# A loop with an empty first pass around the experts' stage of a fused attention, experts and gated-product kernel

## The reference

```python
def attention(q, k, v, f_logit):            # (4, 8, 768, 48)
    f = 1 / (1 + exp(-f_logit))
    for t in range(768):
        state = f[t] * state + outer(k[t], v[t])
        y[t] = q[t] @ state

def experts(x, expert_emb, tau, w1, w2):    # 3072 tokens of 384, 8 experts, width 1024
    logits = unit(x) @ unit(expert_emb).T / tau
    e = argmax(logits, axis=1)
    return softmax(logits)[e] * (relu(x @ w1[e]) @ w2[e])    # per token, one expert

def gated_product(x, w_a, w_b, w_out):      # width 1536
    return ((x @ w_a) * (x @ w_b)) @ w_out
```

## Time and profile before

| | |
|---|---|
| median of 3 runs | 830.19 us (829.87 to 831.49) |
| profiled execution | 830.27 us |
| its span, first to last instruction | 829.0 us |
| TensorE busy | 810.1 us, 98% |
| VectorE, ScalarE, GpSimd busy | 364.4, 321.6, 141.1 us |
| mean granted TensorE clock | 0.995 |

### The profile page before, as it was taken

The page is one execution under the profiler, slowest core; times in us unless marked ns, Lnnn a source line. Parts: engine busy times, 40 slices in busy tenths (PEclk is TensorE's granted clock), DMA queues, the critical chain, the costliest instruction groups (busy, mean ns, idle before and its releaser), DMA issues.

```text
span 829.0 us, 14425 instructions
## 1 busy us (share of the span) xinstructions
PE 810.1 (98%) x5400; PEld 736.9 (89%) x5401; DVE 364.4 (44%) x597; ACT 321.6 (39%) x608; POOL 141.1 (17%) x206
## 2 busy tenths in 40 slices
PE   5999998989999999999999999999999999999998
PEld 4999987989999999998888888888888888888887
DVE  6788877836453645356532322232232223222221
ACT  5677775435453545355421321231222212212211
POOL 4544440423232322100000100010010001001001
PEclk9999999999999999999999999999999999999999
DMA  9777752556552554320000100010010001000001
GB/s 211 194 207 193 201 176 88 110 192 212 206 174 92 207 199 155 125 77 1 0 1 1 39 1 0 1 39 1 0 39 1 1 1 38 1 1 10 28 1 39
DMA packets 32572, 67.57 MB, mean 82 GB/s; under 512 B 12145, under 2 KB 21390, under 8 KB 31374
## 3 DMA queue, kind: packets, MB, share of 16 engines
q1 hardware_dynamic: 28174, 55.93, 22.0%
q0 software_dynamic: 4352, 11.04, 4.3%
HBM read 57.48 MB, written 9.48 MB: 81 GB/s over the span
## 4 chain that ended last, share of the span: by engine, by line
PE 97%; DVE 1%; issue 1%; DMA 0%; ACT 0%; POOL 0%; DVEq 0%
PE low_banks L1024 18%; PE scores L1024 18%; PE sums L1031 9%; PE high_banks L1031 9%; PE sums L978 8%; PE low_banks L967 6%; PE scores L967 6%; PE high_banks L978 4%; PE scores L812 3%; PE sums L828 3%; PE high_banks L801 2%; PE sums L819 2%; PE low_banks L787 2%; PE low_banks L795 1%; PE high_banks L839 1%; PE sums L901 1%
## 5 line engine op out<-in xcount | busy, mean ns | idle before, releaser
L568 POOL DMA_INDIRECT out<-out_sb,placed x24 | 23.3, 970 | 469.3 <-ACT out_sb L758 463.4
L1024 PE MATMUL low_banks<-x_hi,wab_lo 128*128 128x512 f32 x216 | 84.7, 392 | 0.0
L1024 PE MATMUL scores<-x_hi,wab_lo 128*128 128x512 f32 x216 | 84.7, 392 | 0.0
L1024 PE MATMUL low_banks<-yT_lo,wab_hi 128*128 128x512 f32 x216 | 84.6, 392 | 0.0
L1024 PE MATMUL scores<-yT_lo,wab_hi 128*128 128x512 f32 x216 | 84.6, 392 | 0.0
L1024 PE MATMUL low_banks<-x_hi,wab_hi 128*128 128x512 f32 x216 | 84.0, 389 | 0.0
L1024 PE MATMUL scores<-x_hi,wab_hi 128*128 128x512 f32 x216 | 84.0, 389 | 0.0
L1417 DVE TENSOR_TENSOR h<-low_banks,a_sb 128x512 f32<-128x512 f32 x36 | 25.0, 693 | 132.4 <-ACT a_sb L741 132.4
L1417 DVE TENSOR_TENSOR h<-scores,a_sb 128x512 f32<-128x512 f32 x36 | 25.0, 693 | 130.2 <-ACT a_sb L741 117.9
L741 ACT ACTIVATE a_sb<-low_banks 128x512 f32<-128x512 f32 x36 | 21.6, 599 | 137.8 <-PE low_banks L1024 137.8
L741 ACT ACTIVATE a_sb<-scores 128x512 f32<-128x512 f32 x36 | 21.6, 599 | 134.5 <-PE scores L1024 134.5
(11 more groups left out here) (229 smaller groups left out, 1867.8 us busy)
## 6 DMA issues: line engine op xcount, KB each, us to landing
w_raw<-in_w SPq DMA_DIRECT2D x8, 1536.0 KB
w_raw<-in_w SPq DMA_DIRECT2D x32, 384.0 KB
tok<-in_tok SPq DMA_DIRECT2D x48, 192.0 KB, 3.2
qk_all<-in_chan SPq DMA_DIRECT2D x48, 192.0 KB, 3.3
xd<-xst SPq DMA_DIRECT2D x24, 192.0 KB, 1.9
wab_raw<-in_wab SPq DMA_DIRECT2D x6, 768.0 KB, 6.6
wout_raw<-in_wout SPq DMA_DIRECT2D x1, 1536.0 KB, 6.4
wout_raw<-in_wout SPq DMA_DIRECT2D x1, 768.0 KB, 4.3
```

Of the source, the lines that this page charges most:

```text
L568: pool.indirect_dma_start(out=out, out_offset=bass.IndirectOffsetOnAxis(ap=placed[:, u * B + t, 0:1].bitcast(i32), axis=0), in_=out_sb[:, ...
L1024: last_op = pe.matmul(bank[2 * i + m][:, :], w[:, KM * m + k, cols], moving, start=(k == 0 and w is wab_hi and x is not None), stop=(k == ...
```

## The change

The experts' loop on TensorE gets a ninth pass, the first, in which no group is run. The loop starts right behind the rank product; pass 0 jumps over both copies of the group and runs what stood ahead of the loop before: the inversion, the transpose of the table, the 15 `keep_warm` calls, the first group's tiles. The 13 `keep_warm` calls behind the rank product are gone. The surplus body goes behind the loop, with its own transposes.

A narrow group starts when three tiles are there; the fourth is waited for at the fourth column block, whose bank it shares. For a narrow group the fourth tile is not transposed: a matmul of 8 columns counts in its place. TensorE loads the next group's `tile_wide` in the middle of a group to know which. GpSimd waits, before it gathers the fourth tile, for the last landing in it.

VectorE makes 17 of the 24 one-hot tiles. ScalarE makes the other seven, ahead of w1's high half: (low - column) squared, then relu(1 - that). SyncE issues the w2 loads of the first group only when VectorE's first one-hot tile is there.

```diff
+    BY_DVE = 17
...
         sp_eng.wait_ge(ssq_ready, TILES)
+        sp_eng.wait_ge(low_ready, 1)
         for i in range(PAIRS):
             load_w2(slice(0, P), i)
...
                 if j:
                     pool.wait_ge(x1T_done, j * TB - TB + t + 1)
+                    if t == TB - 1:
+                        pool.wait_ge(xin_loaded[t], j * 16)
...
         act.activation(r["norm"][:, :], ssq_all[:, :], ACT.Sqrt).then_inc(norm_ready, 1)
+        act.wait_ge(low_known, 1)
+        for i in range(BY_DVE, TILES):
+            act.activation(off[:, i - BY_DVE, :], column[:, :], ACT.Square, bias=r["low"][:, i:i + 1], scale=-1.0).then_inc(rest_ready, 1)
+        act.wait_ge(rest_ready, TILES - BY_DVE)
+        act.activation(in_low[:, BY_DVE:, :], off[:, :, :], ACT.Relu, bias=1.0, scale=-1.0).then_inc(rest_ready, 1)
         for i in range(PAIRS):
             w1_high(0, i)
...
-        keep_warm(13)
-
-        for i in range(TILES):
-            pe.wait_ge(low_ready, i + 1)
-            last_op = pe.matmul(bank[1][:, 0:TILES], in_low[:, i, :], in_block[:, i, :],
-                                start=(i == 0), stop=(i == TILES - 1))
-        last_op.then_inc(inverted, 1)
...
-        def transpose_x(j, fill=0):
-            for t in range(TB):
...
+        def invert():
+            for i in range(TILES):
+                if i < BY_DVE:
+                    pe.wait_ge(low_ready, i + 1)
+                else:
+                    pe.wait_ge(rest_ready, TILES - BY_DVE + 1)
+                last_op = pe.matmul(bank[1][:, 0:TILES], in_low[:, i, :], in_block[:, i, :],
+                                    start=(i == 0), stop=(i == TILES - 1))
+            last_op.then_inc(inverted, 1)
+            pe.wait_ge(token_ready, 2)
+            pe.wait_ge(x_ready, TILES + 1)
+            pe.transpose(bank[6][0:TILES, 0:P], r["token"][:, :], ident[:, :]).then_inc(tokenT_done, 1)
+            keep_warm(15)
+
+        def transpose_tile(j, t):
+            pe.wait_ge(xin_loaded[t], j * 16 + 16)
+            for k in range(KM):
+                last_op = pe.transpose(bank[t][:, P * k:P * k + P], xin[:, t, P * k:P * k + P], ident[:, :])
+            last_op.then_inc(x1T_done, 1)
+
+        def transpose_fourth(j, wide):
+            with pe.If(wide > 0):
+                transpose_tile(j, TB - 1)
+            with pe.If(wide < 1):
+                pe.matmul(bank[TB - 1][0:32, 0:E], every[:, 0:32], every[:, 0:E], start=True, stop=True).then_inc(x1T_done, 1)
 
         def up(j, n):
             for f in range(FB1):
                 if f % FW == 0:
                     pe.wait_ge(w1l, j * PAIRS + f // FW + 1)
+                if f == TB - 1:
+                    pe.wait_ge(x1l, j * TB + TB)
...
         def group(j, n, i):
+            pe.wait_ge(x1l, j * TB + -(-n // P))
             up(j, n)
+            if i is not None:
+                wide = pe.value_load(tile_wide[0:1, bass.ds(i, 1)], min_val=0, max_val=1)
             pe.wait_ge(y_copied, j * KM + 1)
             down(j, 0, n, True)
-            with pe.If(i < FULL - 1):
-                transpose_x(j + 1)
+            if i is not None:
+                with pe.If(i < FULL):
+                    for t in range(TB - 1):
+                        transpose_tile(j + 1, t)
+                    transpose_fourth(j + 1, wide)
             for m in range(1, KM):
                 down(j, m, n, False)
 
-        transpose_x(0, fill=3)
-        pe.wait_ge(groups_ready, 1)
+        with pe.Fori(0, FULL + 1) as i:
+            with pe.If(i > 0):
+                j = i * (FULL - 1) // FULL
+                chosen = pe.value_load(tile_wide[0:1, bass.ds(j, 1)], min_val=0, max_val=1)
+                with pe.If(chosen < 1):
+                    group(j, 3 * P, i)
+                with pe.If(chosen > 0):
+                    group(j, TW, i)
+            with pe.If(i < 1):
+                invert()
+                for t in range(TB - 1):
+                    transpose_tile(0, t)
+                    keep_warm(3)
+                pe.wait_ge(groups_ready, 1)
+                wide = pe.value_load(tile_wide[0:1, 0:1], min_val=0, max_val=1)
+                transpose_fourth(0, wide)
         more = pe.value_load(tiles_used[0:1, 2:3], min_val=0, max_val=NT - FULL)
         with pe.If(more > 0):
-            with pe.Fori(0, NT - FULL) as j:
-                with pe.If(j < more):
-                    pe.wait_ge(x1l, j * TB + TB)
-                    group(j, TW, 0)
-        with pe.Fori(0, FULL) as i:
-            j = i + more
-            chosen = pe.value_load(tile_wide[0:1, bass.ds(j, 1)], min_val=0, max_val=1)
-            pe.wait_ge(x1l, j * TB + TB)
-            with pe.If(chosen < 1):
-                group(j, 3 * P, i)
-            with pe.If(chosen > 0):
-                group(j, TW, i)
+            with pe.Fori(0, NT - FULL) as extra:
+                with pe.If(extra < more):
+                    for t in range(TB):
+                        transpose_tile(extra + FULL, t)
+                    group(extra + FULL, TW, None)
...
-        link(dve.tensor_copy(r["low"][:, :], place_low[:, :]))
+        dve.tensor_copy(r["low"][:, :], place_low[:, :]).then_inc(low_known, 1)
+        dve.wait_ge(low_known, 1)
...
-        for i in range(TILES):
+        for i in range(BY_DVE):
             dve.tensor_scalar(in_low[:, i, :], column[:, :], r["low"][:, i:i + 1], None, ALU.is_equal).then_inc(low_ready, 1)
```

More of the change, by code:

```diff
@@ L186, in attention_moe_ffn @@
         r[name] = sb("r_" + name, shape)
+    off = sb("off", [P, TILES - BY_DVE, P], f16)
     r["pre"] = sb("r_pre", [P, 1 + E * TILES], f16)
@@ L265, in attention_moe_ffn @@
         sem, ("norm_ready", "ex_ready", "diff_ready", "prefix_ready", "rank_done"))
+    low_known, rest_ready = map(sem, ("low_known", "rest_ready"))
     low_ready, inverted, token_ready, tokenT_done, table_ready, table_stored = map(
```

## The result

The changed kernel took **834.12 us** (median of 6 runs, 833.66 to 835.28) against 830.03 us of the kernel before on the same chip (6 runs, 829.62 to 831.49): a ratio of 1.0046, 95% interval 1.0033 to 1.0059. It is 4.1 us slower, and 826.0 was forecast. The profiled execution has a span of 833.1 us against 829.0, so the traces hold the whole difference.

The account below looks back on a forecast made before the run. TensorE, with 97% of the chain, was taken to bound the kernel. The terms -2.9 - 1.1 - 1.1 + 0.9 = -4.2 us took 830.27 to 826.1, or 826.0 for a median; range 824.2 to 829.3.

Parts of the forecast that it names:

- What bounds the kernel: Whole kernel: TensorE holds 97% of the chain, so only time it loses or works in vain can be won.
- The gap between groups 0 and 1: TensorE's first group boundary: landing code already in store after the empty pass, so the 2.90 us issue gap goes; -2.9 us.
- rival 2: First skip out of group 0 still waits, its block not the one needed or not staying; 829.0 us, chance 0.13.
- The clock: TensorE's granted clock around the inversion: removing 13 keep-warm calls changes nothing, as 30 keep-warm matmuls remain; 0 us.
- The fetch that moves: First jump, now behind the rank product: its wait of at most 4.48 us ends before the inversion needs TensorE; 0 us.
- Inversion: One-hot tiles shared by VectorE and ScalarE ahead of the loop: the token's int copy comes 0.75 us earlier.
- Start of group 0: First expert matmul at 154.1 instead of 155.18, sequencer last, not data; -1.1 us, bounds 0.0 and -1.9.
- Fourth tile: Four narrow groups behind another: three transposes (0.33 us) replaced by a small matmul (0.05); -1.1 us, bounds -1.2 and -0.6.
- Behind the loop: Loop exit: compare, value load and a jump over the never-run surplus body, taken as a miss; +0.9 us, ends 0 and 2.2.
- Slower, the loop no longer stays in store: Experts' loop, longer code: a block fetched anew at each of seven boundaries, 2.9 us each; 846 us, chance 0.05.

Follow-up runs that it names:

- Experiment 1: Changed kernel, but the empty first pass crosses the two copies of the group in two jumps with a landing between them: 829.11 us, ratio 0.9979.
- Experiment 4: 20 keep-warm calls for 15: changed kernel 832.59 us, kernel before 829.13; changed kernel with 17, 24 and 10 calls, one run each: 832.77, 834.23, 832.83.
- experiment 5: Kernel before with 43 never-run instructions and only the one-hot tiles' split between VectorE and ScalarE (with its semaphore): 827.28 us, ratio 0.9957.
- experiment 7: Kernel before, old loop, with never-run padding, the inversion's split and three tiles for narrow groups without the small matmul: 825.42 us, ratio 0.9939.
- Experiment 6: Changed kernel with two jumps in the empty pass, and the third tile's last transpose counting two instead of the small matmul: 826.94 us, ratio 0.9951.
- experiment 3: Kernel before with 43 never-run instructions (ten keep-warm calls under a false condition) behind the inversion: 828.00 us, ratio 0.9967.
- experiment 2: Changed kernel with never-run keep-warm calls inside the loop: 43 instructions 834.09 us, ratio 1.0038; 99 instructions 836.14 us, ratio 1.0058.

## Why the prediction was wrong

**What bounds the kernel: right.** TensorE holds 97% of the chain before and after. The two gaps and the half speed, 0.22 + 1.38 + 2.72 us, make 4.3, a little more than the whole loss of 4.1.

**The gap between groups 0 and 1 (-2.9 forecast, +0.22 measured): wrong, and this is the step that failed.** The step said: the empty pass lands behind both copies, every later skip of the wide copy lands there too, "so it is in store by group 0's end". The landing place is the same, but it was not in store: L1022 waited 4.26 us at 178.1. The reason was argued from a loop whose code had been reached in order ("after one miss the loop's code stayed for seven passes"), and applied to a place reached over a hole of two copies. The fetches fit this: two blocks came up to the middle of group 0, and two more at the boundary, by their time the landing's. Experiment 1 differs in that and a few register instructions, and there the code stays. It was rival 2, with a chance of 0.13 and the right mechanism ("isn't the one needed, or doesn't stay").

**The clock (0 forecast, +2.72 measured): a term that was missing.** I looked for a low clock only at the start, where keep-warm calls were removed. Rival 2 priced the surviving gap as in the kernel before, that is at no change; but a gap of that kind can also cost the clock behind it. With the 2.7, rival 2 would have read 831.7, no longer a gain. The kernel before had its 2.90 us gap at full clock, and I took that for a property of the gap. Experiment 4 shows that it isn't.

**The fetch that moves (0): right.** The first jump out of the rank product waited 3.57 us at 136.8 and ended ahead of the first one-hot at 140.64.

**Inversion (-0.75): right up to the token's copy, then mostly lost.** ScalarE's seven Squares took 2.14 us and the Relu 0.95 (forecast 2.0 and 0.9); from the first one-hot to the token's copy it is 3.41 us against 4.35, so 0.94. But the keep-warm products behind it took longer than before (start us, us, what; the changed kernel, then the one before):

```profile
144.76 5.70 PE sums L912 x30
```

```profile
145.34 5.02 PE sums L901 x30
```

The granted clock was 0.50 until 149.6 against 148.7, so the first tile's transposes came no earlier (150.46 against 150.35). The term for the clock, "so nothing", was wrong here too; the 13 calls taken away are not shown to be the reason, since experiment 5 keeps them and its products took 5.64. The data path, the third x_lo, ended at 154.00 and not at the forecast 153.1.

**Start of group 0 (-1.1): right in size**, 1.10 when counted from the first one-hot, and TensorE waited for nothing that the profile shows in the last 0.45 us, as forecast. But the part of the inversion in it is small: experiment 5 has the inversion without the start on three tiles and gains some 0.4, and experiment 7 adds the start on three tiles and gains 0.9 more. That the sum came out is in part luck: the gather that the working went by was not what TensorE waited for.

**Group 0 itself (0 forecast, +0.30 measured): not foreseen.** One block of 18 took 3.43 instead of 3.12 us. Its first weight load names what it waited for:

```profile
161.00 0.19 PEld L986 LDWEIGHTS low_banks<-x_hi,w_hi 128*128 128x128 f32 x1 [0.36 <-DVE h_lo L1377]
```

This is the fifth column block, which needs a bank back from the first one. VectorE's `h_lo`, which frees it, starts at 160.34 against 160.25 before, though group 0 starts 0.7 us earlier. ScalarE's `h_hi` ahead of it doesn't start earlier either (159.77 against 159.69); what holds that back was not followed. So part of an earlier start is given back there. The wait is also in experiment 7 (3.39) and not in experiment 1 (3.12), where `h_lo` starts at 158.98.

**Fourth tile (-1.1, bounds -1.2 and -0.6; measured 0): the size of one term.** The transposes saved were right at 0.33; the small matmul costs 0.3, not 0.05. Neither end of my range held it, since I took the issue distance of 8-column f16 matmuls in a row for one that stands alone between matmuls of other shapes. Experiment 6 takes it away, and the 0.3 come back.

**Behind the loop (+0.9, bounds 0 and 2.2): right in kind**, 1.38 of gap and 0.26 in the matmuls behind it. The jump took 3.73 us, between the 0.33 and 4.48 of the earlier trace rows. The 0.9 was more than the 0.7 that the working from ScalarE's 2.95 us gave. The Trainium skill ("Runtime: NRT & Kernel Launch", Instruction fetch mechanics) says that a taken jump out of the fetched window stalls; the trace agrees here. Its window of two blocks doesn't fit: groups 2 to 7 jump back over a loop of more than three blocks (by my count of its instructions) without a gap, and no block is fetched from 190 to 360 us.

**Slower, the loop no longer stays in store (846): did not happen.** One boundary had a gap, not seven.

The forecast lay 8.1 us too low: 3.1 from the gap, 2.7 from the clock, 1.1 from the fourth tile, 0.7 at the exit (1.38 and 0.26 against 0.9), 0.3 in group 0 and 0.4 ahead of the change: 8.3.

**What stays open.** Why the block reached over a hole is gone when it is needed again. The runs fit a store that is filled in order, in which the blocks fetched up to the middle of group 0 take its place; no run shows the slots. And what decides between 0 and 2.7 us of slow clock behind a gap.

## What to carry to other kernels

What a jump costs depended here on where its target lay: check the jump's own record, and try a few dozen never-run instructions ahead of it before rewriting a loop for its sake. If a first pass is to bring code into store, let it walk through the blocks in steps, not leap over them. And price a surviving idle stretch on TensorE with the clock behind it, not with its length alone.

## What the runs showed of the hardware

- A jump to code that is not in store took 3.3 to 4.8 us, once 6.63, here with 3 to 4 us of issued matmuls as cover: so a miss shows as a gap of up to 3.5 us, and two in a row as 8.8. Where the fetch had begun ahead of the jump it was 2.16 and 1.81 us (experiments 3 and 4).
- Code behind the two copies, jumped to in one leap, was waited for again 40 us later (4.26 us), with two blocks fetched at that time; with the copies crossed in two jumps, no block was fetched from 144 to 360 us (experiment 1).
- Never-run code made the kernel before 2.7 us faster (experiment 3), and the larger padding made the gap in the changed kernel 8.8 us for 3.12 (experiment 2; span 835.1 against 833.1, with overlapping intervals of the ratios).
- Behind an idle stretch of about 3 us the granted clock was 0.50 until 190.5 in one kernel and full throughout in another; the cost was 0, 1.3, 1.4, 1.6, 2.6 or 2.7 us, and neither the length of the stretch nor its start in the span puts these in order.
- A matmul of 8 columns between float32 transposes and float32 products cost 0.3 us, ten times the 0.03 at which such matmuls follow one another.
